# Attention with a two-part v: two buffers for its halves, and the split moved to the ends of the heads

## The reference

```
B, H, S, D = 4, 8, 576, 64            # 32 heads, block = 64
scores = (q @ k^T) / sqrt(D)          # masked: block of query >= block of key
attn   = exp(scores - rowmax); attn /= rowsum + 1e-9
x      = attn @ v                     # then transposed to (B, S, H*D)
x      = sigmoid(xr @ w_r) * (relu(xk @ w_k)**2 @ w_v)
out    = routed experts: p[e] * relu(x @ w1[e]) @ w2[e], e carried along the tokens by a gate
```

## Time and profile before

| | |
|---|---|
| median of three runs | 770.95 us |
| the profiled execution | 772.05 us |
| its span, first to last instruction | 770.3 us |
| TensorE busy | 741.0 us (96%) |
| VectorE busy | 494.1 us (64%) |
| ScalarE busy | 357.5 us (46%) |
| GpSimd busy | 182.9 us (24%) |
| mean granted TensorE clock | 0.991 |

### The profile page before, as it was taken

One profiled execution on the slowest core, in us unless ns is written; L12 is line 12 of the kernel. 1 busy time (PEld: TensorE's weight loads), 2 busy tenths in 40 slices (PEclk: granted clock), 3 DMA queues, 4 the chain that ended last, 5 costly groups with the idle time before them and its releaser, 6 DMA issues.

```text
span 770.3 us, 13475 instructions
## 1 busy us (share of the span) xinstructions
PE 741.0 (96%) x4054; PEld 661.7 (86%) x4055; DVE 494.1 (64%) x905; ACT 357.5 (46%) x702; POOL 182.9 (24%) x215
## 2 busy tenths in 40 slices
PE   5999999998999999999999999999999999999994
PEld 4888888886989999999999998788888788888882
DVE  8899999996586856859487797622223745453261
ACT  4687877875652606244251432222124644353250
POOL 3345455453200000000020000223323232323231
PEclk9999999998999999999999999999999999999997
DMA  5667676551000010100101071167110176441000
GB/s 158 212 202 224 195 228 190 165 159 43 24 1 1 0 42 1 42 1 1 42 1 43 3 270 42 43 246 274 41 32 27 41 257 235 143 144 40 20 22 8
DMA packets 43063, 74.41 MB, mean 97 GB/s; under 512 B 10061, under 2 KB 20470, under 8 KB 43012
## 3 DMA queue, kind: packets, MB, share of 16 engines
q1 hardware_dynamic: 38676, 64.30, 25.3%
q0 software_dynamic: 4336, 9.47, 3.6%
HBM read 65.31 MB, written 10.57 MB: 99 GB/s over the span
## 4 chain that ended last, share of the span: by engine, by line
PE 83%; DVE 10%; issue 2%; ACT 2%; DMA 1%; ACTq 0%; POOL 0%; POOLq 0%; DVEq 0%
PE ps L841 20%; PE ps L842 20%; PE ps L843 20%; PE ps L779 3%; PE ps L707 2%; PE ps L999 2%; PE ps L733 2%; PE ps L732 2%; PE ps L831 2%; DVE negm L1380 2%; PE ps L710 2%; PE ps L774 1%; DVE sig L1564 1%; PE ps L753 1%; PE ps L908 1%
## 5 line engine op out<-in xcount | busy, mean ns | idle before, releaser
L841 PE MATMUL ps<-we_hi,hT_hi 128*128 (+1 forms) x176 | 73.4, 417 | 2.1 <-DVE o_sb L1856 1.4
L841 PE MATMUL ps<-we_hi,xgT_hi 128*128 (+1 forms) x176 | 70.6, 401 | 0.2 <-DVE xgT_lo L1755 0.2
L1317 ACT ACTIVATE hT_hi<-ps 128x512 fp32r<-128x512 f32 x44 | 26.1, 597 | 94.5 <-PE ps L999 49.4
L842 PE MATMUL ps<-we_lo,xgT_hi 128*128 (+1 forms) x176 | 69.7, 396 | 0.0
L843 PE MATMUL ps<-we_hi,xgT_lo 128*128 (+1 forms) x176 | 69.7, 396 | 0.0
L842 PE MATMUL ps<-we_lo,hT_hi 128*128 (+1 forms) x176 | 69.5, 395 | 0.0
L843 PE MATMUL ps<-we_hi,hT_lo 128*128 (+1 forms) x176 | 69.4, 394 | 0.0
L1151 ACT ACTIVATE pT<-ps 128x256 f32<-128x256 f32 (+2 forms) x192 | 63.1, 388 | 9.3 <-PE ps L733 8.9
L841 PE MATMUL ps<-xm_k_hi,wk_hi 128*128 128x384 f32 x192 | 65.2, 339 | 2.0 <-DVE ksq L1543 1.7
L841 PE MATMUL ps<-ksq_hi,wv_hi 128*128 128x384 f32 x192 | 66.0, 344 | 0.9 <-DVE yT L1578 0.9
L531 POOL TENSOR_TENSOR hi<-qk_raw,hi 64x576 fp32r<-64x576 f32 x32 | 45.2, 1412 | 85.8 <-DVE aug L1407 85.8
(11 more groups left out here) (277 smaller groups left out, 1835.4 us busy)
## 6 DMA issues: line engine op xcount, KB each, us to landing
we_raw<-w SPq DMA_DIRECT2D x12, 2048.0 KB, 11.8
qk_raw<-qkT SPq DMA_DIRECT2D x32, 576.0 KB, 3.9
v_sb<-v SPq DMA_DIRECT2D x16, 320.0 KB, 4.9
inv<-inv_scratch SPq DMA_DIRECT2D x32, 144.0 KB, 4.3
y_scratch<-ytok SPq DMA_DIRECT2D x6, 768.0 KB, 3.5
wk_raw<-w_k SPq DMA_DIRECT2D x8, 256.0 KB, 4.5
wv_raw<-w_v SPq DMA_DIRECT2D x8, 256.0 KB, 4.9
wr_raw<-w_r SPq DMA_DIRECT2D x4, 256.0 KB, 4.8
```

Source lines behind the costliest of these rows:

```text
L841: mm(dst, a_hi, b_hi, start=(k == 0), stop=False)
L842: mm(dst, a_hi, b_lo, start=False, stop=False)
L1317: nc.scalar.activation(hT_hi[:, half * FC // 2:(half + 1) * FC // 2, :].rearrange("p f t -> p (f t)"), ps[:, 3 + half, :], ACT.Copy).then_ ...
```

## The change

`v_hi` and `v_lo` get two buffers each, and pair j uses buffer j % 2, in TensorE's late products too. `split_v` is cut in two. `cast_v(j)` waits for `pv_done` of the pair before the last one and for the load of v, and casts. `split_v(j)` waits for the cast and subtracts. Pair 0 is still cast and subtracted in head 0, in the old place. For the other pairs, the cast of pair i//2 + 1 stands at the end of VectorE's list for the even head i, behind `head_reduce(i+2, 3)`, and the subtraction at the end of that for the odd head. The last pair that is split is 13: its cast stands in head 24 and its subtraction in head 25. GpSimd's first memsets fill both buffers.

```diff
-        v_hi = place("work", "v_hi", [P, 4 * DH], R32)
-        v_lo = place("work", "v_lo", [P, 4 * DH], R32)
+        v_hi = place("work", "v_hi", [P, 2, 4 * DH], R32)
+        v_lo = place("work", "v_lo", [P, 2, 4 * DH], R32)
...
-                nc.gpsimd.memset(v_hi[:, half * DH:half * DH + DH].bitcast(F32), 1.0)
-                nc.gpsimd.memset(v_lo[:, half * DH:half * DH + DH].bitcast(F32), 0.0)
+                nc.gpsimd.memset(v_hi[:, :, half * DH:half * DH + DH].bitcast(F32), 1.0)
+                nc.gpsimd.memset(v_lo[:, :, half * DH:half * DH + DH].bitcast(F32), 0.0)
...
-                mm(end, v_hi[:, cols], p_hi[:, :], start=False, stop=False)
-                mm(end, v_hi[:, cols], pT_lo[:, i % 2, 256:S], start=False, stop=False)
-                mm(end, v_lo[:, cols], p_hi[:, :], start=False, stop=True).then_inc(pv_done, 1)
+                mm(end, v_hi[:, i // 2 % 2, cols], p_hi[:, :], start=False, stop=False)
+                mm(end, v_hi[:, i // 2 % 2, cols], pT_lo[:, i % 2, 256:S], start=False, stop=False)
+                mm(end, v_lo[:, i // 2 % 2, cols], p_hi[:, :], start=False, stop=True).then_inc(pv_done, 1)
...
+            mine = slice(DH, 3 * DH)
+
+            def cast_v(j):
+
+                wait(dve, pv_done, 4 * j - 4)
+                dve.wait_ge(v_loaded[j % 2], 16 * (j // 2) + 16)
+                vec.tensor_copy(v_hi[:, j % 2, mine], v_sb[:, j % 2, 0, mine]).then_inc(v_is_hi, 1)
+
             def split_v(j):
 
-                wait(dve, pv_done, 4 * j)
-                dve.wait_ge(v_loaded[j % 2], 16 * (j // 2) + 16)
-                mine = slice(DH, 3 * DH)
-                vec.tensor_copy(v_hi[:, mine], v_sb[:, j % 2, 0, mine]).then_inc(v_is_hi, 1)
                 dve.wait_ge(v_is_hi, j + 1)
-                vec.tensor_tensor(v_lo[:, mine], v_sb[:, j % 2, 0, mine], v_hi[:, mine].bitcast(F32),
+                vec.tensor_tensor(v_lo[:, j % 2, mine], v_sb[:, j % 2, 0, mine], v_hi[:, j % 2, mine].bitcast(F32),
                                   ALU.subtract).then_inc(v_split, 1)
...
-                if i % 2 == 0 and i < NSPLIT:
-                    split_v(i // 2)
+                if i == 0:
+                    cast_v(0)
+                    split_v(0)
...
                 if i + 2 < NHEAD:
                     head_reduce(i + 2, 3)
+                if i + 2 < NSPLIT:
+                    (cast_v, split_v)[i % 2](i // 2 + 1)
```

## The result

The changed kernel takes 784.0 us (783.59 to 784.94, four runs) against 770.74 us before (769.91 to 771.16, four runs): a ratio of 1.0172, 95% interval 1.0156 to 1.0188. It is slower, by 13.3 us. The forecast was 786.

What follows compares the result with a forecast made beforehand. In the attention TensorE and VectorE were both taken as full; waits for v and smaller terms summed to 15.0 us on the profiled 772.05, giving 787.05 and, with the median 1.10 lower, 786 us (own range 780 to 792; 8 in 10: 779 to 801).

Steps and rivals of the forecast that it cites:

- The step that decides: End of even heads: VectorE reaches the cast at about 5.0 us, v lands at 6.67, so it waits about 1.6.
- The even heads: Even heads 6 to 24: 6.87 us in place of 5.77, 1.10 each, 11.0 us in all.
- GpSimd's share: Casts whose v lands before GpSimd's multiply L540 ends start at 6.50 us: 1 us in all, bounds 0 and 3.
- Nothing is caught up, for neither engine has spare time there: Odd heads behind the wait still take 5.40 us and win back nothing of the delay.
- rival D: TensorE sets the pace and VectorE catches up in odd heads, at most 0.3 us each: 782 us; 66% together with the forecast.
- Where TensorE waits: TensorE's gap moves from L710 of the even head (0.25 to 0.4 us) to L710 of the odd head (about 1.5).
- Rival A: Odd heads 3 to 25: GpSimd's multiply gets in ahead of the subtraction, 1.1 us each, 13 us, so 799 us; 17%.
- Rival B: TensorE's gaps in odd heads lower its clock, about 3.5 us each: 790 to 796 us, 830 if nearly all; 11%.
- The sum: Whole kernel: even heads 11.0, heads 2 and 4 2.9, head 0 0.5, head 26 -0.4, GpSimd 1: 15.0 us.
- Heads 2 and 4: These heads go from 5.40 to 6.87 us, 1.47 each, 2.9 us together.
- a wait in head 0: Head 0 waits for v too, but is long already by its own split: 0.5 us (0 to 1.5).
- The removed work: Front of even heads 6 to 26: cast and subtraction gone, 5.77 to 5.40 us, 11 x 0.37 = 4.1 us.

Runs made afterwards that it cites:

- experiment 2: Changed kernel with the load of v issued ahead of spread_sums, load_row and load_qk: 772.76 us, ratio 1.0018 to the kernel before.
- experiment 6: Changed kernel with the split fifth of v (64 KB) loaded by its own DMA ahead of spread_sums: 768.62 us, ratio 0.9972 to the kernel before.
- 7: Changed kernel without loads of v after the first two pairs, which changes the output: 770.38 us, ratio 0.9991 to the kernel before; total not comparable.
- experiment 4: Changed kernel with the load of v issued behind the weight load of its head: 794.48 us, ratio 1.0280 to the kernel before.
- 1: Changed kernel with cast and subtraction back at the front of the even head, second buffers kept: 771.38 us, ratio 1.0003 to the kernel before.
- the first trace: Profile of the changed kernel in the main measurement: median 784.0 us, ratio 1.0172 to the kernel before.
- 8: The changed kernel run again, unaltered, for a second trace: 781.72 us, ratio 1.0143 to the kernel before.
- experiment 3: Changed kernel with both cast and subtraction of the next pair at the end of the odd head: 776.73 us, ratio 1.0077 to the kernel before.
- experiment 5: Changed kernel with the cast at the end of the odd head, subtraction at the front of the even head: 768.51 us, ratio 0.9961 to the kernel before.
- the earlier trace: Profile of the kernel before the change, which the prediction read: profiled execution 772.05 us, median 770.74 us.

## Why the prediction was right, and where its terms were off

**The step that decides was right: the cast waits for the load of v.** VectorE's idle time stands before L1484, put down to the DMA of v, 1.91 us in the pair shown. Taking away the wait by an earlier load (2), a smaller and earlier one (6) or no load (7) takes away the loss; delaying the load (4) adds to it; the buffers alone (1) do nothing. The load's issue at 1.77 us into the head held (1.75), and so did its landing, 4.9 us in the median in both kernels.

**The even heads** were put at 6.87 us. They came out at 7.08 in the first trace and 6.91 in the second. The size that was off is the landing. From the issue to the start of the cast it was 5.1 us in the mean of the ten heads of the first trace and 4.9 in the second, and up to 6.2 us in head 8 of the first; 5.7 had been the upper bound. GpSimd's share was put at 1 us: two casts began while the multiply ran and took 0.42 and 0.45 us in place of 0.23, 0.4 us in all.

**The step that failed: "Nothing is caught up, for neither engine has spare time there".** Odd heads were put at 5.40 us and take 5.11. That is what rival D foresaw in size, at 0.29 us a head against its 0.3: 2.8 us in ten odd heads of the first trace (5 to 25 without head 9). What I called the whole idle time of VectorE, the round of 0.32, is still there: from the end of the last reduction, 139.99, to `copy_row` at 140.31. So D's reason failed too: the spare time lay in instructions that no row shows as waiting. Before, `head_reduce(·, 0)` began 0.34 us behind `copy_row`, at 122.03 in head 19, just when TensorE's L707 was done (121.53 to 122.00); after a wait for v, TensorE is ahead and it begins after 0.20. And L1415 took 0.67 us, since it began while GpSimd's multiply still ran; now 0.56 (its shape is the same 128x410 in both). 0.14 and about 0.1 are most of the 0.29. The list of waits doesn't show such short ones.

**Where TensorE waits** was half right. I had the whole gap at L710. The row above has 0.54 us at L774, which waits for `copy_row`, and 0.48 at L710.

**Rival A** (GpSimd ahead of the subtraction) did not happen in 12 of 13 subtractions; the other took 0.64 us (head 9, where the clock had fallen: it began 0.94 us behind the multiply). But it is real. In experiment 3 a subtraction 0.18 us or more behind paid 1.1 us in ten odd heads, and a cast or subtraction 0.04 or 0.05 us behind paid it three times in experiment 2 and once each in 5, 6 and 7. This is the Trainium skill's rule (SBUF — State Buffer, "Who interferes with whom"), that the one to issue first holds the shared ports; the traces agree wherever the starts are 0.04 us or more apart. Closer than that the start times don't tell who was first. At the equal start of the earlier trace rows GpSimd had the port, but VectorE kept it three times though its start is written 0.01 us behind the multiply's: twice in experiment 5, and once in experiment 3:

```profile
107.26 1.50 POOL L540 TENSOR_TENSOR xT<-o_raw,inv 64x576 f32<-64x576 f32 x1 [0.20 <-POOL hi L531]
107.27 0.21 DVE L1484 CAST v_hi<-v_sb 128x128 fp32r<-128x128 f32 x1
```

**Rival B** (the clock) came once in the attention: behind the longest wait, 2.9 us before 72.63, the granted clock was 0.50.

```profile
72.00:74.00 2.00, 0.85 (x3) 0.71 (x4) 1.37 (x6) 1.75 (x4) 0.00 (x0) 0.84 0.09 25
74.00:76.00 2.00, 2.00 (x7) 1.51 (x6) 2.00 (x5) 0.47 (x1) 0.06 (x1) 0.50 0.53 112
```

It cost some 1.1 us there, where I had put 3.5 for each fall. TensorE's gap ahead of it was 1.59 us (L774 at 73.14), shorter than the 1.70 of the earlier trace rows that was not followed by a fall, so the length of the gap alone doesn't order them. What I had not thought of is that the clock can also give time back, since the kernel before pays for it as well. Between head 28 and the next layer the traces show three lengths: 25.88 us (before), 25.7 and 25.8 (5, 6), then 24.3 to 24.4 (1, 2, 3, 4, 7, 8), and 22.64 (after). Each trace has one of them.

**The sum.** Put at 15.0 us, measured at 13.3 and 10.9 in the two sessions. By terms of the first trace, up to head 28: even heads 6 to 24 +12.9 (I had 11.0 and 1.0 for GpSimd), odd heads 7 to 25 -1.6 (0), heads 0 to 5 +3.7 (3.4), heads 26 and 27 -0.3 (-0.4), together 14.8; then -3.2 by the clock behind head 28 (0). Heads 2 and 4, with +3.2, came as forecast (2.9). But 0.5 had been put for a wait in head 0; there was none, and the 1.85 us there are TensorE's slow products. Heads 1, 3 and 5 gave 1.3 back (0), 1.0 of it in head 3. So the mechanism of the even heads carried the forecast, and it is luck that the misses around it (+1.4 in head 0, -1.3 and -1.6 in odd heads, -3.2 by the clock) left the total so near.

**The removed work** was worth what I gave it. With the wait gone, the even heads fall to 5.43 to 5.48 us, and the first matmul of the next layer in experiment 6 starts 3.5 us earlier than before (194.12), against 4.1 forecast for that case.

## What to carry to other kernels

Work that is moved into an engine's idle round is free only if its inputs are there: ask when the transfer behind it was issued, and by what. Here the load hung on an instruction of the same head, so that its 4.9 us could not fit before that head's end, and a load of 64 KB ahead of the others turned 13 us of loss into 2 us of gain. Then look at which engine shares a port at the new place; some hundredths of a microsecond decide who waits 1.1 us.

## What the runs showed of the hardware that was not expected

- A gap of TensorE of nearly the same length, 2.22 us before and 2.16 after, was followed by a granted clock of 0.50 in one trace and of 1.00 in the other. At the same place the other eight traces have gaps of 2.14 to 2.24 us, and the clock fell behind each. In experiment 4 one of 1.72 us (ahead of L774 at 65.48) was followed by 1.00, and one of 1.12 (ahead of 78.31) by a fall. The stretch behind head 28 moves by 1.3 to 3.2 us with its clock, as much as the gain of the best version.
- Casting or subtracting 128 columns behind GpSimd's multiply ends with it: 1.44 and 1.41 us in place of 0.21 and 0.29. GpSimd's multiply, in turn, grows from 1.43 to between 1.49 and 1.57 us when it starts up to 0.07 us behind the subtraction; 0.07 us behind the shorter cast it does not grow (1.43 in experiment 3).
- A DMA of 64 KB, issued ahead of the others, landed 2.9 us after its issue (experiment 6), one of 320 KB in the same place after 3.9 (experiment 2, median), and the same 320 KB behind the q and k load after 4.9: in these medians the place in the queue was worth as much as four fifths of the bytes.
